# Moving two q placements and the second weight's loads in the first blocks of an attention + MoE kernel

## The reference

```python
# attention: per chunk of 32 queries, 8 memory keys and a window of 16 + 32 + 8 keys
scores = scale * matmul(q_c, k_full.T); a = exp(scores - max); a = a / (sum(a) + 1e-9)
out[chunk] = matmul(a, v_full)
# first MoE: x is [3072, 512], w_in [512, 1024], w_out [1024, 512]
h = x @ w_in
solu = h * softmax(h)
ln = (solu - mean) / sqrt(var + 1e-6) * g_ln
x2 = ln @ w_out
# second MoE: w_in [512, 2048], w_out [2048, 512]
h = x2 @ w_in; y = maximum(0.01 * h, h) @ w_out
```

## Time and profile before

| | before |
|---|---|
| median of 3 runs | 822.38 us (821.12 to 822.70) |
| the profiled execution | 823.07 us, its span 821.2 us |
| granted TensorE clock, mean | 0.997 |
| TensorE busy | 805.5 us, 98% of the span |
| VectorE busy | 546.6 us, 67% |
| ScalarE busy | 457.7 us, 56% |
| POOL (GpSimd) busy | 98.1 us, 12% |
| DMA, mean over the span | 191 GB/s, 156.64 MB |

### The profile page before, as it was taken

How to read it: one execution, slowest core, us unless ns; L and a number is a source line. 1 busy time by engine, 2 the same in 40 slices (tenths; PEclk the granted TensorE clock), 3 DMA queues, 4 the chain that set the end, 5 groups by cost and what they waited for, 6 DMA issues and landing times.

```text
span 821.2 us, 13098 instructions
## 1 busy us (share of the span) xinstructions
PE 805.5 (98%) x4844; PEld 659.0 (80%) x4844; DVE 546.6 (67%) x906; ACT 457.7 (56%) x737; POOL 98.1 (12%) x220
## 2 busy tenths in 40 slices
PE   8889999999999999999999999999989999999998
PEld 6677778787888888888888888888868888888886
DVE  7778988877743285527643335665788699769775
ACT  4567777767743346345565446566744554555553
POOL 4454445432210000000000000000000000000000
PEclk9999999999999999999999999999999999999999
DMA  9675768665758876246684568445931840373002
GB/s 345 229 274 171 219 197 234 183 191 123 213 198 235 306 264 244 102 174 206 232 289 168 183 221 295 154 155 170 375 145 55 294 166 26 100 266 122 27 1 77
DMA packets 84496, 156.64 MB, mean 191 GB/s; under 512 B 6737, under 2 KB 35537, under 8 KB 84433
## 3 DMA queue, kind: packets, MB, share of 16 engines
q1 hardware_dynamic: 84432, 155.81, 56.6%
HBM read 99.16 MB, written 56.62 MB: 190 GB/s over the span
## 4 chain that ended last, share of the span: by engine, by line
PE 90%; DMA 3%; DVE 2%; issue 1%; POOL 1%; SPq 0%; ACT 0%; POOLq 0%; DVEq 0%
PE hid_a L731 22%; PE hid_b L731 21%; PE attn_ps L731 13%; PE scores_a L731 13%; PE scores_b L731 8%; PE probs_ps L731 7%; PE attn_ps L723 3%; DMA q_raw<-q_in 2%; DMA g_blk<-g_scratch 2%; PE probs_ps L709 2%; PE scores_a L697 1%; PE scores_b L697 1%; DVE ring_lo L1145 1%; DVE g_blk L1293 1%; POOL attn_buf L1435 0%
## 5 line engine op out<-in xcount | busy, mean ns | idle before, releaser
L862 ACT ACTIVATE ring_hi<-g_blk 128x512 fp32r<-128x512 f32 x168 | 105.9, 632 | 111.8 <-PE hid_a L731 42.5
L1145 DVE TENSOR_TENSOR ring_lo<-g_blk,ring_hi 128x512 fp32r<-128x512 f32 x168 | 115.2, 688 | 35.9 <-ACT ring_hi L862 32.6
L1009 ACT ACTIVATE g_out<-g_out 128x512 f32<-128x512 f32 x72 | 45.4, 630 | 71.4 <-DVE g_out L1272 41.1
L731 PE MATMUL hid_b<-ring_hi,w_hi 128*128 128x512 f32 x128 | 49.9, 390 | 0.2 <-DVE ring_lo L1145 0.2
L731 PE MATMUL hid_b<-ring_hi,w_lo 128*128 128x512 f32 x128 | 49.8, 389 | 0.0
L731 PE MATMUL hid_b<-ring_lo,w_hi 128*128 128x512 f32 x128 | 49.8, 389 | 0.0
L731 PE MATMUL hid_a<-w_in_hi,xT_hi 128*128 128x512 f32 x96 | 39.9, 416 | 4.0 <-DVE u L1191 3.3
L1145 DVE TENSOR_TENSOR w_lo<-w_raw,w_hi 128x1792 fp32r<-128x1792 f32 (+2 forms) x24 | 33.6, 1401 | 8.7 <-ACT w_hi L862 8.6
L731 PE MATMUL hid_b<-w_in_hi,xT_hi 128*128 128x512 f32 x96 | 39.3, 409 | 0.0
L1145 DVE TENSOR_TENSOR x_op_P_lo<-op_raw,x_op_P_hi 128x1024 fp32r<-128x1024 f32 x21 | 25.7, 1224 | 19.8 <-ACT x_op_P_hi L862 19.7
L901 ACT ACTIVATE u<-u,shift,gain 128x1024 f32<-128x1024 f32 x24 | 29.8, 1240 | 15.9 <-POOL shift L1455 15.8
(11 more groups left out here) (205 smaller groups left out, 2158.6 us busy)
## 6 DMA issues: line engine op xcount, KB each, us to landing
g_scratch<-g_out SPq DMA_DIRECT2D x96, 256.0 KB, 2.6
g_blk<-g_scratch SPq DMA_DIRECT2D x48, 512.0 KB, 7.2
attn_buf<-k_in SPq DMA_DIRECT2D x32, 384.0 KB, 5.6
attn_buf<-v_in SPq DMA_DIRECT2D x32, 384.0 KB, 3.9
ln_scratch<-lnT SPq DMA_DIRECT2D x24, 512.0 KB, 6.0
w_raw<-w_in SPq DMA_DIRECT2D x16, 512.0 KB, 4.2
q_raw<-q_in SPq DMA_DIRECT2D x32, 192.0 KB, 5.0
ln_even<-ln_scratch SPq DMA_DIRECT2D x12, 512.0 KB, 6.6
```

The source lines that it names most:

```text
L731: mm = pe.matmul(psum, weights[i], data[j], start=first and n == 0, stop=last and n == 2, skip_group_check=goes_on)
L862: return act.activation(dst, src, ACT.Copy)
L1009: act.activation(x, x, ACT.Prelu, alpha=0.01).then_inc(s_g[q], 1)
L1145: return ve.tensor_tensor(dst, x, hi.bitcast(f32), ALU.subtract)
```

## The change

- POOL places q of unit 4 right behind probs(2), and q of unit 5 right behind probs(3); before, both stood behind probs(3) and w1_lo(3) in the list.
- SP issues load_v(4) ahead of load_q(6) and load_k(6).
- The pieces of the second weight are no longer loaded in `START`. Piece t + 3 is loaded at the beginning of block t, for t = 1 to 4, converted by `w1_hi` at that block's end and by `w1_lo` in the block behind it. Before, w1_hi(4) stood at the end of `START`, and w1_lo(4) and w1_hi(5) in block 1.

```diff
-        ("scores", 2), ("load_q", 6), ("load_k", 6), ("place_q", 3),
-        ("values", 0), ("load_v", 4), ("shift", 2),
+        ("scores", 2), ("place_q", 3),
+        ("values", 0), ("load_v", 4), ("load_q", 6), ("load_k", 6), ("shift", 2),
...
-        ("values", 1), ("load_v", 5), ("w1_lo", 1), ("probs", 2),
+        ("values", 1), ("load_v", 5), ("w1_lo", 1), ("probs", 2), ("place_q", 4),
...
-        ("hidden", 1, 1), ("rsum", 3), ("w1_hi", 3), ("x_lo", 2), ("probs", 3),
-        ("hidden", 0, 2), ("w1_lo", 3), ("place_q", 4),
-        ("probs_t", 3), ("place_q", 5),
+        ("hidden", 1, 1), ("rsum", 3), ("w1_hi", 3), ("x_lo", 2), ("probs", 3), ("place_q", 5),
+        ("hidden", 0, 2), ("w1_lo", 3),
+        ("probs_t", 3),
...
-        ("values", 3), ("load_v", 7), ("load_w1", 4), ("rsum", 4),
+        ("values", 3), ("load_v", 7), ("rsum", 4),
...
-        ("values", 4), ("load_v", 8), ("load_w1", 5), ("rsum", 5), ("expo1", 0),
+        ("values", 4), ("load_v", 8), ("rsum", 5), ("expo1", 0),
...
-        ("values", 5), ("load_v", 9), ("load_w1", 6), ("spread", 6),
+        ("values", 5), ("load_v", 9), ("spread", 6),
...
-        ("values", 6), ("load_v", 10), ("shift", 8), ("place_q", 12), ("expo", 8), ("rsum", 8), ("w1_hi", 4), ("probs", 8),
+        ("values", 6), ("load_v", 10), ("shift", 8), ("place_q", 12), ("expo", 8), ("rsum", 8), ("probs", 8),
 )
 BLOCK_STEPS = (
...
-        ("hidden", 1, 0), ("stats", -1), ("w1_lo", 3), ("expo", 6),
+        ("hidden", 1, 0), ("stats", -1), ("w1_lo", 2), ("expo", 6),
...
-        ("values", 6), ("load_v", 10), ("tr", 0), ("probs", 8), ("w1_hi", 4),
+        ("values", 6), ("load_v", 10), ("tr", 0), ("probs", 8), ("w1_hi", 3),
...
     for t in range(1, BLOCKS - 1):
+        if t + KM - 1 < W1_PIECES:
+            add(("load_w1", t + KM - 1))
         for kind, offset, *rest in BLOCK_STEPS:
...
             elif kind in ("w1_hi", "w1_lo"):
-                if t + offset < W1_PIECES:
+                if KM <= t + offset < W1_PIECES:
                     add((kind, t + offset))
-                    if (kind, t + offset) == ("w1_lo", KM):
-                        add(("load_w1", W1_PIECES - 1))
```

## The result

The changed kernel takes **818.56 us** (median of 7, 816.99 to 819.18) against 822.38 (median of 7, 819.62 to 823.13): a ratio of 0.9962, 95% interval 0.9950 to 0.9974. It is faster by 3.8 us; the forecast was 5.06 us. The profiled execution took 816.99 us, the best of its seven, with a span of 815.2.

The account below looks back on a forecast made before the run. TensorE, busy 98% of the span, could win only idle time and slow clock ahead of 64 us. 1.21 + 2.13 + 1.72 = 5.06 us off 822.38 gave 817.3 us, range 815.7 to 820.7.

Parts of the forecast that it names:

- rival B: Clock still falls once, at hidden(2,0) or hidden(4,0), where TensorE idles; price 1.72 us, time 819.0, chance 0.25.
- load_q(6) at 22.6: SP issues load_q(6) at 22.6 instead of 26.31, 3.7 us earlier, because POOL does place_q(4) earlier.
- 1.21 us at hidden(2,0): hidden(2,0) comes 1.21 us earlier: 0.35 from scores(4), and VectorE's gaps of 0.56 and 0.30 closed.
- 2.13 us of waits before and at hidden(4,0): TensorE's waits of 0.18 us before probs_t(8) and 1.95 us before hidden(4,0) both go.
- place_q(12) before 48.3: Deadline on POOL: the copy placing q12 must start by 48.3 instead of 51.68 for hidden(4,0) not to wait.
- The estimate of 4.5 us for the landing: q12's load takes 4.5 us to land, between 3.1 with quiet DMA engines and 6.0 with full ones.
- 1.72 us of slow clock: Twelve matmuls from hidden(4,0) to values(8) took 4.53 us instead of 2.81; the 1.72 us go with the idle time.
- Rival D: Weight pieces ahead of each block's first q delay hidden products, 3.67 us a block; two blocks give 824.7, chance 0.05.
- Rival C: q12 does not count or lands at 51.1; idle time and slow clock at hidden(4,0) stay: 821.2, chance 0.10.

Follow-up runs that it names:

- part 2 alone: Kernel before with the second weight's pieces loaded one a block; q and v as before: 819.25 us, ratio 0.9964.
- piece 4 in front: Changed kernel with piece 4 of the second weight issued right ahead of load_q(12) instead of two loads behind it: 819.80 us, ratio 0.9967.
- part 1 alone: Kernel before with q of units 4 and 5 placed earlier and v4 ahead of q6; second weight's pieces as before: 820.11 us, ratio 0.9980.
- the kernel before with the fill: Kernel before with 7 small matmuls, result unread, in TensorE's idle time before hidden(4,0): 821.00 us against 822.59, ratio 0.9983.
- the changed one with six: Changed kernel with 6 small matmuls in TensorE's idle time before hidden(2,0): 818.02 us, the second time 817.93 us.
- solu(0) sooner: Changed kernel with VectorE's and ScalarE's order around hidden(2,0) changed, solu(0) right behind rsum(6), and probs(6) ahead of place_q(8): 818.83 us, ratio 0.9960.

## Why the prediction was right, and where it was off

The direction, the place and the chain of waits held; one term of the sum did not. The median of 818.56 lies 1.26 us above the 817.3 forecast, inside the range, and it is nearer to rival B's 819.0.

- **load_q(6) at 22.6**: it was 21.55, since q4 landed sooner in this execution. That v4 stood ahead of q6 changed nothing that the run without it can show. The step took the DMA engines to run empty when v4 goes out; they were full (1.03 of the time from 16.83 to 21.55 us): v4 and k5 took 7.0 us each to land, and both were still under way when q6 was issued.
- **1.21 us at hidden(2,0)**: the profile has 1.48. VectorE and TensorE moved together as the step said, with the rest given back as idle time, 1.57 us where 1.65 was forecast.
- **2.13 us of waits before and at hidden(4,0)**: both went. Counted from the same point, hidden(4,0) came 3.86 us earlier, against 3.34 from the two terms: the extra is 0.27 us at hidden(2,0) and 0.25 us between there and hidden(4,0), which was not followed further. It is luck in the sum: without it the two terms alone would have given 819.0. And the part of it that scores(6) lost varies between executions of the same code, as part 2 alone shows.
- **place_q(12) before 48.3**: 47.7 on the footing of before, 0.6 us early. The estimate of 4.5 us for the landing was near: 4.8, 5.3 and 3.6 us in three profiles. The margin is as thin as the prediction had it, and the run with piece 4 in front shows that the deadline is real.
- **1.72 us of slow clock**: this is the term that was wrong. One fall costs that much TensorE work, 1.7 us in each of the eight profiles that have one (the missing share of the clock times the length, in tables by 2 us), and filling the idle time in the kernel before won 1.6 us. But its worth in the difference of the medians was not 1.72 us. I read it from one profiled execution that had lost it and took it as lost in each, while 22 of 56 executions of the kernel before have no fall at all; and I gave rival B a chance of 0.25 as if the clock fell either always or never. It falls in a part of the executions of both kernels, 34 of 56 and 11 of 21. Nor does it fall wherever TensorE idles near 1.65 us, as rival B read the rule: with 1.56 to 1.58 us it fell in four of eight profiles. B's mechanism came true in a part of the executions, and its time is the nearest. The mean of the clocks is 0.9984 in both, so in the sum this term is near 0. What the idle times gave is 3.86 us in one pair of profiles, and the medians differ by 3.82.
- **Rival D** fell: TensorE is busy 146.00 of 146.00 us from 64 to 210 us with the pieces in blocks 1 to 4. **Rival C** fell by the runs of the single parts and by piece 4 ahead of q12.

That the clock fell at hidden(2,0) in the kernels of part 1 alone, of part 2 alone, of v4 back behind q6 and of piece 4 first, and in none of the three profiles of the changed kernel, I take for chance: all have 1.57 or 1.58 us of idling there, and the kernel with piece 4 first differs from the changed one only in a load that goes out behind the fall. Where the clock falls in the executions that were not profiled was not seen. The profiles show three places: hidden(4,0) in the kernel before, hidden(2,0) in kernels with a part of the change or an edit to it, and the border to the last product in three kernels of the study (the kernel before with the fill, the changed one with six, and solu(0) sooner). How the 34 and the 11 executions with a fall divide among them stays open.

## What to carry to other kernels

Read what each queue waits for before asking what it carries: one copy of 1 us, placed behind the wrong step on POOL, left SP's queue without an issue for 10 us, and every later load of q late. A cost that hangs on the clock has to be weighed by how many executions pay it, which one profile cannot tell; the clocks listed for many executions can, but not where it was paid: for that look through the whole span of each profile, and not only at the place that was changed. And an idle time that is moved can take the clock's risk with it.

## What the runs showed of the hardware

- The same idle time can cost the clock or not. Eight profiles, the filled kernel before among them, have 1.56 to 1.58 us of idling before hidden(2,0), behind work that filled TensorE for 7.04 to 7.88 of the 8 us from 29 to 37 us; in four of them the granted clock then goes to its lower level of 1.2 GHz for some 3 us (0.52 from 39 to 42 us with part 1 alone), in four it stays at 2.4 GHz. In the four profiles with the fill there it never fell at that place. At the border to the last product it fell behind 2.40, 2.44 and 2.46 us of idling and stayed up behind 2.38. The Trainium skill, "TensorE: Matmul & The Clock Gate" (What's actually happening), says that the moment at which the clock changes is not tied to the kernel's start and varies from run to run. The page speaks of when; here it is whether the fall happens at all that varies, which fits it.
- A load of 192 KB of q took 3.4 us from issue to landing with k5 and v4 still under way (q6, the DMA engines busy 0.89 of that time), and 4.8, 5.3 and 3.6 us (q12, in the three profiles of the changed kernel) with them busy 0.83, 0.83 and 0.77 of the time from the issue to the copy. So the busy share alone does not tell how long a single load takes.
- The 20 small matmuls of the opening, the first work that TensorE does, took 3.92 us in the profile of the kernel before and 4.64 us in that of the changed one, with the same code. Two profiles of this kernel can differ by 0.7 us from this alone.
